# Tokens by parity, a PSUM bank each for even and odd ones, in a fused recurrence and two gated layers

## The reference

```python
for t in range(S):
    cur = np.einsum('bhd,bhe->bhde', u[None] * kt, vt)
    y[:, :, t] = np.einsum('bhd,bhde->bhe', rt, state + cur)
    state = wt[:, :, :, None] * state + np.einsum('bhd,bhe->bhde', kt, vt)
```

## Time and profile before

| | us |
|---|---|
| median of 3 runs (lowest to highest) | 417.6 (416.84 to 419.27) |
| the profiled execution | 420.01 |
| its span, first to last instruction | 418.3 |
| PE busy | 364.8 (87%) |
| DVE busy | 253.9 (61%) |
| ACT busy | 190.4 (46%) |
| POOL busy | 120.9 (29%) |

### The profile page before, as it was taken

How to read it: one execution, slowest core, us unless ns; L and a number is a source line. 1 busy time by engine, 2 the same in 40 slices (tenths; PEclk the granted TensorE clock), 3 DMA queues, 4 the chain that set the end, 5 groups by cost and what they waited for, 6 DMA issues and landing times.

```text
span 418.3 us, 9108 instructions
## 1 busy us (share of the span) xinstructions
PE 364.8 (87%) x3836; PEld 344.8 (82%) x3836; DVE 253.9 (61%) x384; ACT 190.4 (46%) x326; POOL 120.9 (29%) x138
## 2 busy tenths in 40 slices
PE   5665868978878698668999999999999999999997
PEld 4554657767768586568998999999999999999996
DVE  6357867687979967650655445998796311764011
ACT  4435626666774645533312416627783700565100
POOL 6705524346447343000000000610970000463000
PEclk9998958989999999969999999999999999999999
DMA  8986670606202110101000001306000011000011
GB/s 161 233 199 134 177 175 3 133 15 141 60 4 60 30 30 2 30 2 49 19 2 0 0 2 26 126 0 196 15 2 0 2 40 55 19 2 0 19 39 56
DMA packets 58584, 23.59 MB, mean 56 GB/s; under 512 B 52656, under 2 KB 56112, under 8 KB 58544
## 3 DMA queue, kind: packets, MB, share of 16 engines
q1 hardware_dynamic: 58544, 23.02, 21.8%
HBM read 18.29 MB, written 2.36 MB: 49 GB/s over the span
## 4 chain that ended last, share of the span: by engine, by line
PE 78%; issue 7%; ACT 7%; DVE 6%; DVEq 0%; ACTq 0%
PE ps L1184 20%; PE ps L1186 19%; PE ps L1185 19%; PE ps L1175 5%; PE ps L1107 5%; PE ps L1171 3%; PE ps L1140 2%; PE ps L1129 2%; ACT r L617 1%; DVE kT L860 1%; PE ps L1117 1%; ACT rU L615 1%; PE ps L1145 1%; ACT ktok L639 1%; ACT yT L672 1%
## 5 line engine op out<-in xcount | busy, mean ns | idle before, releaser
L552 POOL TENSOR_TENSOR r<-r,wb 112x768 f32<-112x768 f32 x24 | 41.3, 1732 | 83.9 <-PE ps L1175 83.9
L599 POOL TENSOR_TENSOR sq_f<-sq_f 128x384 f32<-128x384 f32 x32 | 33.8, 1071 | 74.9 <-ACT sq_f L742 74.8
L860 DVE TENSOR_TENSOR kT<-kT,wb 112x384 f32<-112x384 f32 x40 | 35.0, 876 | 18.7 <-PE ps L1175 18.5
L1027 DVE TENSOR_TENSOR ot<-ps,ee 128x384 f32<-128x384 f32 x12 | 6.7, 557 | 54.6 <-PE ps L1186 54.6
L1175 PEld LDWEIGHTS ps<-r,kT 112*64 112x64 f32 x960 | 34.3, 150 | 5.8 <-issue 3.8
L1175 PE MATMUL ps<-r,kT 112*64 112x64 f32 x960 | 38.7, 238 | 0.4 <-issue 0.2
L1012 DVE TENSOR_TENSOR sq_l<-sq_f,sq_h 128x384 fp32r<-128x384 f32 x32 | 27.7, 864 | 10.3 <-ACT sq_h L747 10.3
L1186 PE MATMUL ps<-xk_h,wk_l 128*128 128x384 f32 x96 | 32.2, 335 | 0.0
L1185 PE MATMUL ps<-xk_l,wk_h 128*128 128x384 f32 x96 | 32.2, 335 | 0.0
L1184 PE MATMUL ps<-xk_h,wk_h 128*128 128x384 f32 x96 | 32.2, 335 | 0.0
L1184 PE MATMUL ps<-wv_h,sq_h 128*128 128x384 f32 x96 | 32.1, 334 | 0.0
(11 more groups left out here) (148 smaller groups left out, 969.9 us busy)
## 6 DMA issues: line engine op xcount, KB each, us to landing
tok_w<-in_w_dram SPq DMA_DIRECT2D x16, 144.0 KB, 3.0
...
```

The source lines that it names most:

```text
L552: nc.gpsimd.tensor_tensor(t, t, pair_of(h, 0, q).unsqueeze(1).unsqueeze(3).broadcast_to([ROWS, 2, S // (2 * h), h]), ALU.mult).then_inc(r_ ...
L599: nc.gpsimd.tensor_tensor(t, t, t, ALU.mult).then_inc(k_sq, 1)
L860: nc.vector.tensor_tensor(t, t, pair_of(h, 1, q).unsqueeze(2).broadcast_to([ROWS, S // (2 * h), h]), ALU.mult).then_inc(k_scaled, 1)
```

## The change

The tokens are loaded so that a transpose puts the even ones in one bank of `turn` and the odd ones in the other. ACT and DVE then read whole banks instead of every second column, `first_k` waits for the even half of `kU` alone and `first_r` for the odd half of `rU`, and the decays of level 0 lie as two halves. v is loaded into two zero-padded halves (`vt` doubles, POOL zeroes it, four DMAs for two), and `ktok` is one copy. `wsg_h` is written straight from PSUM and `wsg_l` is subtracted from PSUM at once (`low_sg`), so that k now waits for it too; the six ACT splits and the six late `low_half` go. The jobs of the slots are written in another order for PE, ACT and DVE. `w_sg` is loaded into a ring of three.

```diff
-            jobs = [("kt", a - 3), ("level", a - 2, 4), ("w", a + 1), ("level", a - 1, 2), ("sg", a - 2), ("level", a, 0),
+            jobs = [("level", a - 2, 4), ("kt", a - 3), ("w", a + 1), ("level", a - 1, 2), ("sg", a - 2), ("level", a, 0),
                     ("k", a + 1), ("u", a - 3)]
         else:
-            jobs = [("level", a - 2, 5), ("level", a - 1, 3), ("r", a + 1), ("level", a, 1), ("y", a - 3)]
+            jobs = [("level", a - 2, 5), ("r", a + 1), ("level", a - 1, 3), ("level", a, 1), ("y", a - 3)]
...
+        if slot % 2 == 0:
+            jobs = [("kt", a - 3), ("w", a + 1), ("wm", a - 3), ("sg", a - 2), ("k", a + 1), ("sy", a - 3)]
+        else:
+            jobs = [("r", a + 1), ("y", a - 3)]
...
     SPLITS = {2: ("in", 0), 3: ("in", 1), 4: ("in", 2), 5: ("in", 3), 6: ("in", 4), 7: ("in", 5),
-              8: ("sg", 0), 9: ("sg", 1), 10: ("sg", 2), 11: ("sg", 3), 13: ("sg", 4), 14: ("sg", 5),
               15: ("out", 0), 16: ("out", 1), 17: ("out", 2)}
-    LOW_SLOTS = [3, 4, 5, 6, 7, 8, 14, 15, 16, 17, 18, 19, 20, 20, 21]
+    LOW_SLOTS = [3, 4, 5, 6, 7, 8, 20, 20, 21]
...
+            vt[s] = under(f"vt{s}", [P, 2, C, ROWS], F32)
...
         def pair_of(h, parity, q):
+            if h == 1:
+                return wT[0:ROWS, parity * HF:(parity + 1) * HF]
             return blocks(q, h).rearrange("p (n two) -> p n two", two=2)[:, :, parity]
...
-                        sp.dma_start(tok[s][kind][:, :, 64 * x:64 * x + D],
-                                     src[b, 2 * p + x].rearrange("(c p) d -> p c d", p=P)
+                        sp.dma_start(tok[s][kind][:, :, 64 * x:64 * x + D].rearrange("p (two c) d -> p two c d", two=2),
+                                     src[b, 2 * p + x].rearrange("(c p two) d -> p two c d", p=P, two=2)
...
-                    sp.wait_ge(zeroed, VT_ZEROED)
+                    sp.wait_ge(late_zeroed, VT_ZEROED + q)
+                    for g in range(2):
+                        sp.dma_start(vt[q % 4][CHUNK[g], g, :, 64 * x:64 * x + D],
+                                     v[b, 2 * p + x].rearrange("(c g p) d -> g p c d", g=2, p=CH)[g]
+                                     ).then_inc(v_in[q % 4], 16)
...
+            for s in range(4):
+                nc.gpsimd.memset(vt[s][:, :, :, :], 0.0).then_inc(late_zeroed, 1)
...
-                        to, found = by_parity(in_banks(rU[lo:hi, x, :])), by_parity(src[lo:hi, :, 0:HF])
-                        nc.scalar.activation(to[:, 0], found[:, 0], ACT.Copy, scale=ucol[lo:hi, q % PPB:q % PPB + 1])
-                        nc.scalar.copy(to[:, 1], found[:, 1])
+                        ins = nc.scalar.copy(by_parity(rU[lo:hi, x, :])[:, 1], src[lo:hi, 1, 0:HF])
+                    ins.then_inc(r_odd_out, 1)
                     for x, (lo, hi) in enumerate(HEADS):
-                        ins = nc.scalar.copy(by_parity(in_banks(r2[q % 5][lo:hi, x, :]))[:, 0],
-                                             by_parity(src[lo:hi, :, 0:HF])[:, 0])
+                        nc.scalar.activation(by_parity(rU[lo:hi, x, :])[:, 0], src[lo:hi, 0, 0:HF], ACT.Copy,
+                                             scale=ucol[lo:hi, q % PPB:q % PPB + 1])
+                    for x, (lo, hi) in enumerate(HEADS):
+                        ins = nc.scalar.copy(by_parity(r2[q % 5][lo:hi, x, :])[:, 0], src[lo:hi, 0, 0:HF])
                     ins.then_inc(copied, 1)
                 elif kind == "k":
...
-                    to, found = by_parity(in_banks(kU[0:ROWS, :])), by_parity(src[0:ROWS, :, 0:HF])
-                    nc.scalar.copy(to[:, 0], found[:, 0])
-                    nc.scalar.activation(to[:, 1], found[:, 1], ACT.Copy, scale=ucol[0:ROWS, q % PPB:q % PPB + 1])
-                    nc.scalar.copy(by_parity(in_banks(kT[q % 4][0:ROWS, :]))[:, 1], found[:, 1]).then_inc(copied, 1)
+                    to = by_parity(kU[0:ROWS, :])
+                    nc.scalar.copy(to[:, 0], src[0:ROWS, 0, 0:HF]).then_inc(k_even_out, 1)
+                    nc.scalar.activation(to[:, 1], src[0:ROWS, 1, 0:HF], ACT.Copy, scale=ucol[0:ROWS, q % PPB:q % PPB + 1])
+                    nc.scalar.copy(by_parity(kT[q % 4][0:ROWS, :])[:, 1], src[0:ROWS, 1, 0:HF]).then_inc(copied, 1)
...
-                    for g in range(2):
-                        ins = nc.scalar.copy(ktok[CHUNK[g], g, :, :].rearrange("p (b c) x -> p b c x", b=2),
-                                             src[CHUNK[g], :, 0:3 * ROWS].rearrange("p b (c x) -> p b c x", c=3))
-                    ins.then_inc(copied, 1)
+                    nc.scalar.copy(ktok[:, :, :].rearrange("p (b c) x -> p b c x", b=2),
+                                   src[:, :, 0:3 * ROWS].rearrange("p b (c x) -> p b c x", c=3)).then_inc(copied, 1)
                 else:
-                    nc.scalar.copy(wsg_f[:, :, q * P:(q + 1) * P].rearrange("p (b j) t -> p b j t", b=2),
+                    nc.scalar.copy(wsg_h[:, :, q * P:(q + 1) * P].rearrange("p (b j) t -> p b j t", b=2),
...
+                    act.wait_ge(turned, turn_at[("kt", 5)] + 1)
+                    act.wait_ge(mixed, 7 if n >= 6 else 5)
...
+                for job in act_jobs(slot):
+                    elif job[0] == "wm":
                         spread_products(job[1])
+                    elif job[0] == "sy":
+                        lay_states(job[1])
                     else:
...
-                dve.wait_ge(copied, turn_at[("k", q)] + 1)
+                dve.wait_ge(copied, turn_at[("w", q)] + 1)
+                dve.wait_ge(k_even_out, q + 1)
...
+                nc.vector.tensor_tensor(by_parity(kT[q % 4][0:ROWS, :])[:, 0], turn_banks(("k", q))[0:ROWS, 0, 0:HF],
+                                        pair_of(1, 1, q), ALU.mult).then_inc(k_scaled, 1)
...
+            def low_sg(n):
+
+                dve.wait_ge(copied, turn_at[("sg", n)] + 1)
+                c = slice(n * P, (n + 1) * P)
+                nc.vector.tensor_tensor(wsg_l[:, :, c].rearrange("p (b j) t -> p b j t", b=2),
+                                        turn[:, :, 0:HF].rearrange("p b (j t) -> p b j t", j=3),
+                                        wsg_h[:, :, c].bitcast(F32).rearrange("p (b j) t -> p b j t", b=2),
+                                        ALU.subtract).then_inc(sg_low, 1)
...
-                for job in side_jobs(slot - 1) if slot else []:
+                for job in pe_jobs(slot):
+                    if job[0] == "level":
+                        q, l = job[1:]
+                        if l:
+                            scale_k(q, l)
+                        if 0 < l < DVE_R:
+                            scale_r(q, l)
+                        take_level(q, l)
+                    elif job[0] == "sg":
+                        low_sg(job[1])
...
+                    elif job[0] == "u":
+                        chain(job[1])
...
+                elif last[0] == "sg":
+                    pe.wait_ge(sg_low, last[1] + 1)
```

More of the change, by code:

```diff
@@ L63, in side_jobs, with act_jobs @@
         return [job for job in pe_jobs(slot) if job[0] != "level"]
+    def act_jobs(slot):
+        a = slot // 2
+        if slot % 2 == 0:
+            jobs = [("kt", a - 3), ("w", a + 1), ("wm", a - 3), ("sg", a - 2), ("k", a + 1), ("sy", a - 3)]
+        else:
+            jobs = [("r", a + 1), ("y", a - 3)]
+        jobs = [job for job in jobs if 0 <= job[1] < (C if job[0] == "sg" else NP)]
+        return jobs + EARLY_DENSE.get(slot, [])
     EARLY_DENSE = {16: [("V", 0, 0), ("V", 0, 1)], 17: [("V", 0, 2), ("V", 0, 3)], 18: [("V", 0, 4), ("V", 0, 5)],
@@ L81, in rwkv_gmlp_channel_mix_kernel @@
     for slot in range(SLOTS):
[L82 to L85, removed]
+        K_SCALES += [(q, l) for q, l in level_jobs(slot) if l] + [(q, 0) for kind, q, *_ in side_jobs(slot) if kind == "k"]
         R_SCALES += [(q, l) for q, l in level_jobs(slot) if 0 < l < DVE_R]
+        R_SCALES += [(q, 0) for kind, q, *_ in side_jobs(slot) if kind == "r"]
     POOL_SCALES = [(q, l) for q, l in LEVEL_JOBS if l >= DVE_R]
@@ L222, in rwkv_gmlp_channel_mix_kernel @@
         wm = under("wm", [P, D, SCAN], F32)
-        ktok = under("ktok", [P, 2, C, ROWS], F32)
+        ktok = under("ktok", [P, C, ROWS], F32)
         wb = [under(f"wb{s}", [P, S], F32) for s in range(2)]
@@ L366, in blocks @@
         def blocks(q, h):
-            if h == 1:
-                return wT[0:ROWS, :]
             if h == CH:
@@ L381, in by_parity @@
         def by_parity(t):
-            return t.rearrange("d b (n two) -> d two b n", two=2)
+            return t.rearrange("d (n two) -> d two n", two=2)
         def in_banks(t):
@@ L472, in _ @@
             load_pair(4)
-            for t in range(2, C):
-                load_sg(t)
+            load_sg(2)
             load_v(1)
@@ L573, in _ @@
                 nc.gpsimd.memset(wchunk[s][:, :], 0.0).then_inc(wc_zeroed, 1)
-            for z in (sy[:, :, D:CH], ktok[:, :, :, :]):
-                nc.gpsimd.memset(z, 0.0).then_inc(late_zeroed, 1)
```

(25 more changed lines are left out.)

65 lines of the change are left out of this document (26 added, 39 removed).

## The result

The changed kernel takes 423.6 us (median of 4 runs, the lowest 422.52), the kernel before 418.2 beside it: ratio 1.0123 [1.0078, 1.0168]. It is slower, where 410.3 was forecast. The profiled execution took 422.52 (span 420.8); by span against span it is +2.5 us, where the sum said -7.3.

What follows compares the result with a forecast made beforehand. DVE's chain from scan to `first_r` was taken to bound a turn. The terms -0.5 - 1.9 - 1.3 + 0.4 - 1.6 - 2.5 - 0.9 + 1.0 gave -7.3, 412.7 us, scaled to 410.3; own range 407 to 413, wider range 403 to 416.

Steps and rivals of the forecast that it cites:

- What bounds the kernel: In a turn, w to w: DVE's chain from scan to end of `first_r` (8.9 us) is the bound.
- The steady turn, 16.3: Turn without slow clock: 15.94 - 0.1 up to the scan + 0.5 behind it, so no gain (+0.4).
- 17.3, if POOL's level 4 scaling, now released before kt, also gets ahead of DVE's level 1: Upper bound of the steady turn, with one more 1.0 us of DVE waiting for POOL.
- The charge for the clock, +1.0 in all: PE's waits gather ahead of w, about 2.5 us; a slow w, level 2 and sg delay the scan 1.4 us.
- The clock rival: The gap ahead of w slows PE in each of three turns, 3 x 1.4 us, giving 413; chance 0.2.
- Pair 5's turn, -1.3: From 17.58 us to the steady 16.3, as the slow clock behind the wait for r goes.
- Pair 4's turn: From 20.42 us to 18.5, -1.9: the slow start stays, the second slow stretch behind r goes.
- To w of pair 4, -0.5: Stretch before 56.45 us: earlier `first_k` and moved `low_half` against added `low_sg`; between -2 and +1.
- w of pair 7 to dense, -1.6: Up to the first dense matmul, two old `low_half` (1.27 each) leave DVE's chain, one `low_sg` (1.0) enters.
- The late terms, -3.4: Late slots: -2.5 from `sy` ahead of the gelus, -0.9 from `ktok` in one copy.
- `low_sg`, 1.0 us: DVE's subtraction from PSUM ahead of k, taken at 1.0 us, between 0.96 and 1.27; k starts 0.6 later.
- The slower rival: `low_sg` holds k, gaps keep PE at 1.2 GHz through whole turns; 425 us; chance 0.08.

Runs made afterwards that it cites:

- e11: Changed kernel with PE's old slot order in both places and the six `low_half` of win in odd slots 3 to 13; 413.87 us, ratio to before 0.9891.
- e13: Changed kernel with its orders, plus one wait: POOL's level 4 scaling waits for DVE's r-scaling for level 1 of the next pair; 418.48 us, ratio 0.9990.
- e7: e1 with `first_k` and `first_r` put back behind `chain`, so `first_k` follows the scan; 420.14 us, ratio to before 0.9975.
- e12: e11 with 56 (pair 4) and 20 (from pair 5) filler matmuls ahead of w's transposes; 414.96 us, ratio to before 0.9881.
- e1: Changed kernel with PE's old slot order in both places (kt ahead of level 4, level 3 ahead of r); 417.60 us, ratio to before 0.9966.
- e5: e1 with 110 (pair 4), then 48 extra matmuls ahead of w's transposes; 419.12 us, ratio to before 0.9972.
- e6: Changed kernel with 110 (pair 4), then 60 extra matmuls ahead of w's transposes; 423.28 us, ratio to before 1.0090.
- e8: e1 with the old `wsg_f`, ACT splits and late `low_half` in place of `low_sg`; 420.81 us, ratio to before 1.0039.
- e10: Kernel before with only the copy to `sy` moved ahead of the dense gelus of its slot on ACT; 415.22 us, ratio 0.9915.

## Why the prediction was wrong

**What bounds the kernel: right.** The cycle w, k, u, scan, DVE's chain, `first_r`, w held in every kernel, and what shortened the chain (e11, e13) shortened the time. One part was not as thought: `first_k` out of the chain (-0.46) gave it nothing, since the first L863 then waits longer for POOL (e7).

**The steady turn, 16.3: near as a size at full clock, wrong as the turn of this kernel.** e12 gives 16.4, in part by luck: its chain is 9.1 us where 9.4 was worked out (the three collisions cost 0.7, 0.9 and 0.8 us, 2.4 and not 2.85), and its way to the scan is 7.2 where 6.8 was, since a `low_half` now stands ahead of the levels there. The step that failed is the choice among the bounds: "17.3, if POOL's level 4 scaling, now released before kt, also gets ahead of DVE's level 1". It was on the page as a bound of one turn and got no chance of its own; the sum took three collisions, the kernel had four. It was worth 5.6 us of time (e13), not one. The profiled executions show 1.3 us of chain in the turns of pairs 6 and 7, and a wait ahead of w of 3.3 us instead of 1.1, behind which w, level 2 and sg run slow and the scan comes 8.8 us after w instead of 6.9 (pair 7, changed kernel against e1). That the two could meet was to be read from the order of the jobs, since level 4's scores end one transposing step earlier; which of them comes first is a matter of 0.14 us in the trace, so it needed a chance of its own.

**The charge for the clock, +1.0 in all: mis-sized.** From w to the scan the three turns take 8.7, 8.9 and 8.25 us, where 6.9 is the way at full clock (e5, e6). Pair 4's was in the sum, so 2.0 and 1.3 for the other two, and 1.9 for pair 7, are 5.2 us where 1.0 was charged. The clock rival said 3 x 1.4, which is near, and had 0.2. It and the fourth collision came together, and behind the longer wait (3.28 us) w, level 2 and sg all ran at 1.2 GHz; the rivals were priced as if only one could come. In the changed kernel w or sg ran at 1.2 GHz behind each wait of 2.1 to 4.2 us ahead of w. With the warning of the Trainium skill on waits that recur between bursts ("TensorE: Matmul & The Clock Gate", section "HAM oscillation — how this bites in real kernels") this trace agrees, more than the +1.0 did.

**Pair 5's turn, -1.3: wrong.** It was taken as the steady turn, but slot 8 keeps its `low_half` between the scan and level 5 (chain 10.12): +0.7 against 9.4, and 2.1 on the way to the scan (8.9 against 6.8). Together 2.8, as measured.

**Pair 4's turn: right in size** (18.9 for 18.5), with the chain 0.7 longer than worked out and the scan 0.4 sooner.

**To w of pair 4, -0.5: +0.6.** Within the bounds of -2 to +1; the kernels with this body reach it at 57.0 to 60.6, so it isn't told apart from the scatter of executions.

**w of pair 7 to dense, -1.6: near in size, the mechanism only in part.** e1 has 31.8 where 31.4 was worked out; the changed kernel has 35.1 through the two effects above. But e8, with the two old `low_half` back, has 32.2, so the exchange is worth 0.5 us up to there: two `low_sg` stand in the stretch and not one, and the three subtractions of `x_l` take 4.02 us in e1 and 2.77 in e8. What made up the rest of the 33.0 of before is not shown.

**The late terms, -3.4: right.** -3.0 measured, -2.3 for `sy` alone in e10, and the wait of u behind the norm is 6.22 us, 0.7 less.

**`low_sg`, 1.0 us: right** (957 ns). The row of the take that also reads PSUM priced it, not that of the old L916, and its effect on k is an idle 0.47 us ahead of k's transposes, 0.6 taken.

**The slower rival: not it.** PE was not at 1.2 GHz through whole turns (mean clocks 0.85 to 0.88). The time was slower by a cause that stood only among the bounds, and by a clock that was charged too little.
